# Feed-forward layer 0: the numerator as a product on VectorE and a line on ScalarE, summed by an adding DMA

## The reference

```python
x = attn_out laid out as 3072 tokens x 384       # a delta-rule attention, not touched here
# layer 0
h = x @ w_in                                     # 384 -> 2048
P = a[0] + a[1] * h + a[2] * h**2 + a[3] * h**3  # the numerator
Q = 1.0 + abs(b[0]) * abs(h) + abs(b[1]) * h**2
g = P / (Q + 1e-06)
x = g @ w_out                                    # 2048 -> 384
# layer 1: the same two products, g = h * tanh(log(1 + exp(min(h, 20))))
```

## Time and profile before

| what | us |
|---|---|
| median of 3 executions | 1152.55 (1148.77 to 1155.8) |
| the profiled execution, its own time | 1156.6 |
| its span, first to last instruction | 1154.8 |
| TensorE busy in the span | 1039.5 (90%) |
| VectorE busy | 935.9 (81%) |
| ScalarE busy | 727.5 (63%) |
| GpSimd busy | 185.2 (16%), none of it in the feed-forward part |

### The profile page before, as it was taken

How to read it: one execution, slowest core, us unless ns; L and a number is a source line. 1 busy time by engine, 2 the same in 40 slices (tenths; PEclk the granted TensorE clock), 3 DMA queues, 4 the chain that set the end, 5 groups by cost and what they waited for, 6 DMA issues and landing times.

```text
span 1154.8 us, 24086 instructions
## 1 busy us (share of the span) xinstructions
PE 1039.5 (90%) x10274; PEld 823.8 (71%) x10280; DVE 935.9 (81%) x996; ACT 727.5 (63%) x943; POOL 185.2 (16%) x332
## 2 busy tenths in 40 slices
PE   4487788988888999999999999899999999999997
PEld 2365565766666777777877778678888888888886
DVE  4965555456399999999999999999788887878785
ACT  1133434455487787777868778777766767667664
POOL 5088886582000000000000000000000000000000
PEclk6579989799899999999999999999999999999999
DMA  7823434223300010100101002240100101010000
GB/s 173 234 58 99 112 100 126 60 71 113 111 28 28 1 55 1 55 0 0 54 0 55 1 18 96 79 136 1 43 12 1 55 0 54 0 55 1 28 1 28
DMA packets 28192, 61.82 MB, mean 54 GB/s; under 512 B 3648, under 2 KB 11328, under 8 KB 28096
## 3 DMA queue, kind: packets, MB, share of 16 engines
q1 hardware_dynamic: 27584, 59.13, 17.0%
q10 hardware_dynamic: 512, 1.31, 0.5%
HBM read 46.27 MB, written 14.16 MB: 52 GB/s over the span
## 4 chain that ended last, share of the span: by engine, by line
DVE 35%; PE 34%; issue 3%; ACT 2%; DVEq 0%; ACTq 0%
PE o_ps L838 6%; PE o_ps L840 6%; PE o_ps L839 6%; PE h_ps L839 6%; PE h_ps L838 6%; PE h_ps L840 6%; DVE val L1023 5%; DVE val L1042 5%; DVE val L1055 5%; DVE g_lo L1061 5%; DVE den L1015 5%; DVE den L1050 5%; DVE pa L1021 5%; PE h_ps L882 0%; ACT den L902 0%
## 5 line engine op out<-in xcount | busy, mean ns | idle before, releaser
L911 ACT ACTIVATE g_hi<-val 128x1024 fp32r<-128x1024 f32 x96 | 102.0, 1062 | 100.1 <-DVE val L1055 94.0
L838 PE MATMUL o_ps<-g_hi,w_hi_late 128*128 128x512 f32 x288 | 116.7, 405 | 20.8 <-DVE g_lo L1061 20.7
L1055 DVE SCALAR_TENSOR_TENSOR val<-den,val 128x1024 f32<-128x1024 f32 x96 | 117.7, 1226 | 10.3
L838 PE MATMUL o_ps<-g_hi,w_hi_early 128*128 128x512 f32 x288 | 114.5, 398 | 12.8 <-ACT stage L948 9.2
L1061 DVE SCALAR_TENSOR_TENSOR g_lo<-val,g_hi 128x1024 fp32r<-128x1024 f32 x96 | 117.6, 1225 | 1.6 <-ACT g_hi L911 1.5
L838 PE MATMUL h_ps<-x_hi,w_hi_early 128*128 128x512 f32 x288 | 112.9, 392 | 2.0 <-DVE val L1023 2.0
L838 PE MATMUL h_ps<-x_hi,w_hi_late 128*128 128x512 f32 x288 | 112.5, 391 | 1.6 <-DVE w_lo_late L87 1.6
L839 PE MATMUL o_ps<-g_lo,w_hi_late 128*128 128x512 f32 x288 | 113.5, 394 | 0.0
L840 PE MATMUL o_ps<-g_hi,w_lo_early 128*128 128x512 f32 x288 | 113.4, 394 | 0.0
L840 PE MATMUL o_ps<-g_hi,w_lo_late 128*128 128x512 f32 x288 | 113.3, 394 | 0.0
L839 PE MATMUL o_ps<-g_lo,w_hi_early 128*128 128x512 f32 x288 | 113.3, 393 | 0.0
(11 more groups left out here) (114 smaller groups left out, 2226.3 us busy)
## 6 DMA issues: line engine op xcount, KB each, us to landing
w_raw<-w SPq DMA_DIRECT2D x16, 768.0 KB, 5.0
kv_run<-kv_n SPq DMA_DIRECT2D x24, 384.0 KB, 3.7
x_raw<-x_dram SPq DMA_DIRECT2D x12, 768.0 KB, 5.7
kq<-kq_t SPq DMA_DIRECT2D x44, 192.0 KB, 5.1
x_dram<-stage SPq DMA_DIRECT2D x12, 384.0 KB, 4.3
x_dram<-stage SPq DMA_DIRECT2D x6, 768.0 KB, 4.2
out<-stage SPq DMA_DIRECT2D x5, 768.0 KB, 4.1
k_norm<-kv_n SPq DMA_DIRECT2D x4, 768.0 KB, 7.3
```

The source lines that it names most:

```text
L838: nc.tensor.matmul(dst, hi, rhs_hi, start=first, stop=False)
L911: act_fn(g_hi[:, n % 2], val[:, n % 2], ACT.Copy, scale=-1.0).then_inc(g_hi_ready, 1)
L1055: dve_stt(val[:, e], den[:, e], 2.0, val[:, e], ALU.subtract, ALU.mult).then_inc(g_ready, 1)
```

## The change

Layer 0 writes P as (a3*h + a2)*h^2 + (a1*h + a0). ScalarE makes the two lines (`pa`, and now `val`), VectorE makes the product `pa*sq` (`cubic`), and a DMA that GpSimd issues adds `pa` to `val`, both of 128x1024 float32 (512 KB) in SBUF. VectorE's two instructions of `above` are gone, `cubic` is new, and `ratio` becomes a plain product that waits for the adding DMA (`num_added`). The first instruction of `corrected` becomes `unit` and stands before `ratio`. `h_ps` is now read by ScalarE alone, and `h_read` is signalled by its fourth instruction of `front`. The second line of `front` waits for `g_lo_ready` of the step before last, since it writes `val`.

```diff
--- before.py
+++ after.py
@@ -775,10 +775,12 @@
         x_loaded = hand.x_loaded
         x_hi_ready, x_lo_ready = sem("x_hi_ready"), sem("x_lo_ready")
         h_done, h_read = sem("h_done"), sem("h_read")
-        abs_ready, lead_ready = sem("abs_ready"), sem("lead_ready")
+        line_ready, lead_ready = sem("line_ready"), sem("lead_ready")
+        cubic_ready, num_added = sem("cubic_ready"), sem("num_added")
+        pool_passed = sem("pool_passed")
         exp_ready, clip_ready, one_ready = sem("exp_ready"), sem("clip_ready"), sem("one_ready")
         q_ready, ln_ready, rec_ready = sem("q_ready"), sem("ln_ready"), sem("rec_ready")
-        inner_ready, ratio_ready, unit_ready = sem("inner_ready"), sem("ratio_ready"), sem("unit_ready")
+        ratio_ready, unit_ready = sem("ratio_ready"), sem("unit_ready")
         g_ready = sem("g_ready")
         g_hi_ready, g_lo_ready, g_used = sem("g_hi_ready"), sem("g_lo_ready"), sem("g_used")
         o_done, o_copied, o_stored = sem("o_done"), sem("o_copied"), sem("o_stored")
@@ -832,6 +834,20 @@
                 sp.dma_start(features(out[:, T - 1])[:, m], o_stage[:, m]).then_inc(o_stored, 16)
             sp.wait_ge(o_stored, 16 * (2 * T + KT))
 
+        @block.gpsimd
+        def _(pool):
+            def numerator(dt, n):
+
+                e = n % 2
+                pool.wait_ge(line_ready, DT * dt + n + 1)
+                pool.wait_ge(cubic_ready, DT * dt + n + 1)
+                pool.sem_inc(pool_passed, 1)
+                nc.gpsimd.dma_start(val[:, e], pa[:, e], accum_op=ALU.add).then_inc(num_added, 16)
+
+            with pool.Fori(0, T // 2) as dt:
+                for n in range(DT):
+                    numerator(dt, n)
+
         @block.tensor
         def _(pe):
             def three(dst, hi, lo, rhs_hi, rhs_lo, first, last):
@@ -893,14 +909,18 @@
         def _(act):
             act_fn = nc.scalar.activation
 
-            def front(layer, dt, n):
+            def front(layer, dt, n, warm=True):
                 e = n % 2
                 act.wait_ge(h_done, DT * dt + n + 1)
                 h = h_ps[e][:]
                 if layer == 0:
                     act_fn(sq[:, e], h, ACT.Square)
-                    act_fn(den[:, e], h, ACT.Abs, scale=cf[:, 4:5]).then_inc(abs_ready, 1)
                     act_fn(pa[:, e], h, ACT.Identity, scale=cf[:, 3:4], bias=cf[:, 2:3]).then_inc(lead_ready, 1)
+                    if warm:
+
+                        act.wait_ge(g_lo_ready, DT * dt + n - 1)
+                    act_fn(val[:, e], h, ACT.Identity, scale=cf[:, 1:2], bias=cf[:, 0:1]).then_inc(line_ready, 1)
+                    act_fn(den[:, e], h, ACT.Abs, scale=cf[:, 4:5]).then_inc(h_read, 1)
                 else:
                     act_fn(den[:, e], h, ACT.Exp).then_inc(exp_ready, 1)
 
@@ -959,7 +979,7 @@
                 for n in range(DT):
                     following = layer if n + 1 < DT else after
                     if following is not None:
-                        front(following, dt, n + 1)
+                        front(following, dt, n + 1, not (first and n == 0))
                     if following == 1:
                         squared(dt, n + 1)
                         logarithm(1, dt, n + 1)
@@ -987,7 +1007,7 @@
             act.wait_ge(coef_loaded, 16)
             act_fn(cf[:, 6:7], cf[:, 5:6], ACT.Abs).then_inc(coef_made, 1)
             act.wait_ge(coef_made, 2)
-            front(0, 0, 0)
+            front(0, 0, 0, False)
             logarithm(0, 0, 0)
             reciprocal(0, 0)
 
@@ -1011,16 +1031,14 @@
             def below(dt, n):
 
                 e = n % 2
-                dve.wait_ge(abs_ready, DT * dt + n + 1)
+                dve.wait_ge(h_read, DT * dt + n + 1 + 2)
                 dve_stt(den[:, e], sq[:, e], cf[:, 6:7], den[:, e], ALU.mult, ALU.add).then_inc(q_ready, 1)
 
-            def above(dt, n):
+            def cubic(dt, n):
 
                 e = n % 2
                 dve.wait_ge(lead_ready, DT * dt + n + 1)
-                dve_tt(pa[:, e], pa[:, e], h_ps[e][:], ALU.mult).then_inc(inner_ready, 1)
-                dve.wait_ge(inner_ready, DT * dt + n + 1)
-                dve_stt(val[:, e], pa[:, e], cf[:, 1:2], h_ps[e][:], ALU.add, ALU.mult).then_inc(h_read, 1)
+                dve_tt(pa[:, e], pa[:, e], sq[:, e], ALU.mult).then_inc(cubic_ready, 1)
 
             def clipped(dt, n):
                 e = n % 2
@@ -1037,19 +1055,24 @@
 
                 e = n % 2
                 dve.wait_ge(rec_ready, DT * dt + n + 1)
-                dve.wait_ge(h_read, DT * dt + n + 1 + 2)
                 if layer == 0:
-                    dve_stt(val[:, e], val[:, e], cf[:, 0:1], rec[:, e], ALU.add, ALU.mult).then_inc(ratio_ready, 1)
+                    dve.wait_ge(num_added, 16 * DT * dt + 16 * n + 16)
                 else:
-                    dve_tt(val[:, e], val[:, e], rec[:, e], ALU.mult).then_inc(ratio_ready, 1)
-
-            def corrected(layer, dt, n):
-
-                e = n % 2
+                    dve.wait_ge(h_read, DT * dt + n + 1 + 2)
+                dve_tt(val[:, e], val[:, e], rec[:, e], ALU.mult).then_inc(ratio_ready, 1)
+
+            def unit(layer, dt, n):
+
+                e = n % 2
+                dve.wait_ge(rec_ready, DT * dt + n + 1)
                 if layer == 0:
                     dve_stt(den[:, e], den[:, e], ONE, rec[:, e], ALU.add, ALU.mult).then_inc(unit_ready, 1)
                 else:
                     dve_stt(den[:, e], sq[:, e], 1.0, rec[:, e], ALU.add, ALU.mult).then_inc(unit_ready, 1)
+
+            def corrected(dt, n):
+
+                e = n % 2
                 dve.wait_ge(ratio_ready, DT * dt + n + 1)
                 dve.wait_ge(unit_ready, DT * dt + n + 1)
                 dve_stt(val[:, e], den[:, e], 2.0, val[:, e], ALU.subtract, ALU.mult).then_inc(g_ready, 1)
@@ -1068,14 +1091,22 @@
 
                 for n in range(DT):
                     following = layer if n + 1 < DT else after
-                    ratio(layer, dt, n)
-                    if following == 1:
-                        clipped(dt, n + 1)
-                    corrected(layer, dt, n)
+                    if layer == 0:
+                        unit(layer, dt, n)
+                        ratio(layer, dt, n)
+                        if following == 0:
+                            cubic(dt, n + 1)
+                        else:
+                            clipped(dt, n + 1)
+                    else:
+                        ratio(layer, dt, n)
+                        if following == 1:
+                            clipped(dt, n + 1)
+                        unit(layer, dt, n)
+                    corrected(dt, n)
                     if following == 0:
                         below(dt, n + 1)
                         low_part(dt, n)
-                        above(dt, n + 1)
                     elif following == 1:
                         mish_above(dt, n + 1)
                         low_part(dt, n)
@@ -1095,8 +1126,8 @@
             nc.vector.memset(shifts[:, 1:2], 1.0).then_inc(coef_made, 1)
             split(0, 0)
             dve.wait_ge(coef_made, 2)
+            cubic(0, 0)
             below(0, 0)
-            above(0, 0)
             two_tiles(0, 0, 0, LATE)
             with dve.Fori(1, T // 2 - 1) as dt:
                 two_tiles(0, dt, 0)
```

## The result

The changed kernel takes 1141.91 us (median of 9 runs, 1133.81 to 1143.11) against 1152.55 before (9 runs, 1146.94 to 1158.51): a ratio of 0.990 with a 95% interval of 0.987 to 0.992, which is 9 to 15 us (the quotient of the two medians is 0.991). The profiled execution takes 1137.16 us, its span is 1135.4; busy are TensorE 1029.8 us (91%), VectorE 869.6 (77%), ScalarE 779.8 (69%), GpSimd 227.7 (20%).

A forecast was written before the change was run, and what follows sets the result against it. VectorE was taken to bound layer 0 and TensorE layer 1. The terms -21.6 + 2.5 + 3.9 + 5 gave -10.2 us, from 1156.6 to 1146.4 profiled, or 1142 from the median; range 1133 to 1192, the forecast's own 1133 to 1147.

The forecast's parts named there:

- plain steps: Layer 0's steps without extra work: from 8.67 to 8.21 us, 47 x 0.46 = -21.6 us.
- extras: Layer 0's tile copies and splits of x and weights, now in the loop: 22 us against 19.5 before, +2.5 us.
- start of the layer: Layer 0's first steps: `below(0)` waits for four ScalarE instructions instead of two, `below(1)` comes at 329.0, +3.9 us.
- late DMAs: Layer 0, once a tile: the adding DMA lands behind the store and load of x; 1 us five times, +5 us.
- copies: ScalarE's copies of a finished tile stand ahead of sq, so `cubic` starts 1.16 us later, 5 times.
- x_hi: ScalarE's part of the split of x in layer 0: +1.1 us, 6 times.
- x_lo: VectorE's part of the split of x in layer 0, behind g_lo: +0.4 us, 6 times.
- L: Layer 0: time from the end of VectorE's product to the adding DMA's semaphore; taken as 5.1 us, with 5.86 allowed.
- the rival: Layer 0: the adding DMA takes longer than 5.86 us and becomes the bound, slower than before; 1193 at 7.5; chance 0.37.
- The collisions: Layer 0's adding DMA behind each tile's store and load of x: 1 us, 5 times, +5 us, 0 to +10.
- Rival 2: Layer 0: a tie, the DMA taking 6.0 to 6.6 us or GpSimd held up by VectorE; 1147 to 1158 us; chance 0.12.
- Rival 3: Tile boundaries: TensorE's wait for the copies costs +3 us and its low clock +3; ends at 1148; chance 0.08.

The follow-up runs named there:

- e7: Changed kernel without the first instruction of layer 0's Newton correction (`unit`), so its result is wrong; plain step 7.88 to 8.17 us, one run, 1129.81 us.
- e2: Changed kernel with `pa` added to `val` twice, one adding DMA behind the other; plain step 12.65 us, one run, 1354.17 us.
- e3: Changed kernel with `ratio` put ahead of `unit` again; plain step 8.70 us, ratio 1.007 to the kernel before.
- e5: Changed kernel with the first two loads of layer 1's weights issued some 300 us earlier; ratio 0.988 to the kernel before.
- e6: As e5, with the split of x cut into three pieces on each engine, put into three steps; 1128.35 us, ratio 0.979 to the kernel before.

## Why the prediction was right

Forecast 1142, measured 1141.91; the mechanism was the forecast one. But the agreement of the total is partly luck: the measured interval alone leaves 9 to 15 us, and two terms were off by more than 2 us in opposite directions. Its terms against the trace, up to `below` of the last step:

| term | forecast | measured |
|---|---|---|
| plain steps | -21.6 | 46 x (8.14 - 8.67) = -24.4 |
| extras | +2.5 | 25.1 - 20.2 = +5.0 |
| start of the layer | +3.9 | 13.51 - 9.65 = +3.9 |
| late DMAs | +5 | 0.86 + 4.88 = +5.7 |
| sum | -10.2 | -9.8 |

- **Plain steps, mis-sized.** The chain through VectorE and ScalarE was put at 8.17 and measured 8.14. I took TensorE's 8.21 as the floor above it, from layer 1's mean over 47 steps. Layer 1's steps are 8.16 but for its first three (9.30, 9.66 and 7.71), which the mean had in it; e7 shows 8.15 for layer 0.
- **Extras, mis-sized by the same error.** Each was right by itself: copies +1.20 (forecast 1.16), x_hi +1.11 (1.1), x_lo +0.43 (0.4). The first two follow from e7's loop through pa: the x_hi split puts 1.38 more between exp and sq (412.69 to 415.04 in the trace, 2.35 instead of 0.97), and 7.88 + 1.38 = 9.26. The sum was 25.1 against my 23.9, since weight steps that also split x cost 2.1 to 2.5; and the old kernel's extras were 20.2, not 19.5. The rest is the 1.9 us that I let the plain steps make good, which did not come: with both bounds within 0.02 us there is no lead to make good from.
- **The start** came out as worked, step by step: `below(1)` 13.51 us after the first sq, 9.65 before.
- **The adding DMA**: L forecast 5.1, measured 5.2 (0.56 to the issue, 4.6 to the landing), by trace and again by e2 and e3. The way there was not right in its parts: plain 512 KB land in 2.9 us (3.1 by the rows), the add takes 1.7 more (2.0), and the 0.56 was not in the estimate at all. A margin of 0.6 us held on an unmeasured part, so the chance of 0.37 for the rival was fair: e3 shows what 1.14 us would have done.
- **The collisions**: right in size, wrong in place. The store and load of x, which I charged with 1 us five times, make it land after 4.9, 5.0 and 5.0 us in three tiles, which the room of 0.6 us hides, and after 6.0 in the fourth, which lengthens the step by 0.86; 4.9 us come in the fifth, where two weight loads stand behind them (3.3 of it by e5's steps), which I did not list. With the weight loads gone that DMA still lands after 6.7 us (e5).
- **Rival 2**, GpSimd held up by VectorE: not seen. The landing time has a minimum of 4.5 and a median of 4.6 beside a VectorE that is 85% busy, the issue stands 0.56 to 0.58 us behind the product in 47 of 48 steps, and it keeps GpSimd for 0.86 us there as well as in e2's second issue, most of which falls into VectorE's idle time. This agrees with the rule quoted there from the Trainium skill (SBUF — State Buffer, who interferes with whom). My estimate from the Trainium skill in the prediction, 4.4 us (DMA: Bandwidth & Descriptors, anatomy of a DMA on the GpSimd path; Collectives: The Full Stack, why the reducing step runs at half the pace), is 0.2 below the 4.6 from issue to landing.
- **Rival 3**: TensorE does wait for the copies (6.1 us over five tiles), but the loop is late in those steps anyway by 1.2. Of the low clock that I charged twice, layer 0 shows one stretch at granted clock 0.50 once its start is over, about 690 to 693 us, behind the longest wait for the DMA, in which TensorE had stood idle (no matmul from 686 to 688); the tile boundaries before it have 1.00 (329 to 688 us).
- **ScalarE** was to be near 85% busy and is 92%. The prediction's own rows say more than 85: 52.53 of 70 us at 8.67 us a step is 6.5 us, and one more instruction of 1.21 in 8.2 us makes 94%.
- **Layer 1** was to keep its time; it got 2.1 us shorter, most of it in its first step, and the attention's end moved by 7.5 us with no edit. As a sign, equal times of these parts were too sharp for a single profile.

## What to carry to other kernels

Lay the loop out in time before the edit, engine by engine with start-to-start slots: that gave the loop of VectorE and ScalarE to 0.03 us. Lay out the second-longest loop too: it says how much of an addition is hidden (8.14 - 7.88 = 0.26 us here). Then look for holes: work that sits outside them lengthens the loop by all that exceeds this, and the same work cut to the hole's size is free (e6). Moving an operation to a DMA is worth what the hole on its old engine is worth, no more, and its latency must fit the room between producer and user, which the order of two neighbouring instructions moves by a slot (1.14 us here, where 0.6 is spare). A floor taken from another stage's mean carries that stage's exceptions with it; take it from its plain step.

## What the runs showed that I had not expected

An adding DMA of 512 KB from GpSimd within SBUF lands 4.5 to 4.6 us after its issue in 42 of 48 cases, and 10.0 after it behind 3 MB of other transfers. The plain copy takes 2.9. GpSimd is busy 0.86 and 0.53 us an issue. The attention part, unchanged, ended at times 11.6 us apart in twelve profiles, which is more than the whole effect of this change: what a change does is read from the stretch that it touches.
